# A fused attention and two-layer MoE kernel on one core: logits with the weights held, output additions spread, last pairs' steps in order of tiles, new banks and queues at the start of the second MoE

## The reference

```python
# attention: B=2, H=8, S=576, D=64; the 32 largest scores of each row count
scores = scale * q @ k.T
mask = scores >= kth_largest(scores, 32)
x = softmax(where(mask, scores, -1e9)) @ v          # 1152 tokens x 512
# first MoE: E=8 experts, F=1024, all experts on all tokens, Sinkhorn gates
P = exp(x @ w_gate - max)
for _ in range(8):
    P /= P.sum(1); P /= P.sum(0); P *= N / E
out = sum(P[:, e:e+1] * (relu(x @ w1[e]) @ w2[e]) for e in range(8))
# second MoE, dense: F=2048
h = out @ w_in
g = h * tanh(softplus(h))
result = g @ w_out
```

## Time and profile before

| | |
|---|---|
| three runs | 1254.61, 1255.6, 1258.02 us |
| median | 1255.6 us |
| profiled execution | 1254.9 us, span 1252.8 us |
| granted TensorE clock, mean | 0.985 |
| PE busy | 1202.7 us, 96% |
| DVE busy | 894.3 us, 71% |
| ACT, POOL busy | 685.1 us, 643.1 us |
| DMA | 112 MB, 89 GB/s |

### The profile page before, as it was taken

One profiled execution on the slowest core, in us unless ns is written; L12 is line 12 of the kernel. 1 busy time (PEld: TensorE's weight loads), 2 busy tenths in 40 slices (PEclk: granted clock), 3 DMA queues, 4 the chain that ended last, 5 costly groups with the idle time before them and its releaser, 6 DMA issues.

```text
span 1252.8 us, 19662 instructions
## 1 busy us (share of the span) xinstructions
PE 1202.7 (96%) x6715; PEld 1073.9 (86%) x6715; DVE 894.3 (71%) x1556; ACT 685.1 (55%) x1223; POOL 643.1 (51%) x393
## 2 busy tenths in 40 slices
PE   4878999999999999999999999999999998999998
PEld 4777889999999999998878888888888887898776
DVE  6999998899999940356575464646464647887876
ACT  5667776676777753442243333333333336878776
POOL 1867865556665567753487666666666630000000
PEclk8699999999999999999999999999999999999999
DMA  9034332233223322332233222222222122222230
GB/s 168 9 100 144 120 102 92 94 109 102 94 92 110 110 89 98 118 113 81 68 106 105 68 92 67 90 69 85 74 77 81 44 76 68 68 68 85 85 126 34
DMA packets 150486, 112.10 MB, mean 89 GB/s; under 512 B 34832, under 2 KB 124944, under 8 KB 150416
## 3 DMA queue, kind: packets, MB, share of 16 engines
q1 hardware_dynamic: 150416, 111.19, 29.2%
HBM read 104.09 MB, written 7.08 MB: 89 GB/s over the span
## 4 chain that ended last, share of the span: by engine, by line
PE 78%; DVE 11%; ACT 7%; issue 2%; POOL 1%; DMA 0%; DVEq 0%; SPq 0%; POOLq 0%; ACTq 0%
PE ps L725 15%; PE ps L897 15%; PE ps L739 14%; PE ps L958 14%; PE ps L634 4%; PE ps L1075 4%; PE ps L1053 4%; PE ps L605 3%; PE ps L615 2%; DVE work L1461 2%; DVE top L1459 2%; ACT m_r L1393 1%; ACT m_d L1390 1%; PE ps L594 1%; ACT m_r L1395 1%
## 5 line engine op out<-in xcount | busy, mean ns | idle before, releaser
L1858 POOL TENSOR_TENSOR w_lo<-w_raw,w_hi 128x1024 fp32r<-128x1024 f32 x90 | 218.7, 2431 | 117.4 <-ACT w_hi L1105 117.3
L1105 ACT ACTIVATE w_hi<-w_raw 128x1024 fp32r<-128x1024 f32 (+1 forms) x172 | 179.4, 1044 | 1.6 <-PE ps L897 1.0
L1459 DVE MAX8 top<-work 128x8 f32<-128x576 f32 x216 | 152.2, 745 | 0.0
L725 PE MATMUL ps<-x_hi,w_hi 128*128 128x384 f32 (+3 forms) x384 | 129.5, 337 | 1.7 <-DVE h_lo L1572 1.7
L725 PE MATMUL ps<-x_hi,w_lo 128*128 128x384 f32 (+3 forms) x384 | 128.7, 335 | 0.0
L725 PE MATMUL ps<-x_lo,w_hi 128*128 128x384 f32 (+3 forms) x384 | 128.5, 335 | 0.0
L1865 POOL TENSOR_TENSOR ha_lo<-h_f,ha_hi 128x384 fp32r<-128x384 f32 (+1 forms) x72 | 71.9, 998 | 93.9 <-ACT ha_hi L1182 93.9
L897 PE MATMUL ps<-w_hi,h_lo 128*128 128x512 f32 x296 | 117.2, 396 | 0.0
L897 PE MATMUL ps<-w_lo,h_hi 128*128 128x512 f32 x296 | 117.0, 395 | 0.0
L897 PE MATMUL ps<-w_hi,h_hi 128*128 128x512 f32 x296 | 115.2, 389 | 0.0
L1461 DVE MATCH_REPLACE8 work<-top,work 128x576 f32<-128x576 f32 x144 | 105.7, 741 | 0.0
(11 more groups left out here) (183 smaller groups left out, 3292.4 us busy)
## 6 DMA issues: line engine op xcount, KB each, us to landing
w_raw<-in_moe_w SPq DMA_DIRECT2D x288, 256.0 KB, 3.0
w_raw<-in_moe_w_in SPq DMA_DIRECT2D x32, 256.0 KB, 2.7
w_raw<-in_moe_w_out SPq DMA_DIRECT2D x32, 256.0 KB, 3.0
spill<-y_out SPq DMA_DIRECT2D x5, 768.0 KB, 3.8
y_in<-spill SPq DMA_DIRECT2D x5, 768.0 KB, 4.4
q_parts<-in_q SPq DMA_DIRECT2D x18, 128.0 KB, 3.2
vones<-in_v SPq DMA_DIRECT2D x8, 256.0 KB, 4.9
out<-acc SPq DMA_DIRECT2D x8, 256.0 KB, 2.6
```

Source lines behind the costliest of these rows:

```text
L725: last = nc.tensor.matmul(ps[:, bank, 0:w], wt[:, s, 0, c * P:(c + 1) * P], xt[:, c, token:token + w], start=(n == 0), stop=(n == len(term ...
L1105: return nc.scalar.activation(dst, src, ACT.Copy)
L1459: last = v_.max(top[:, b, op // 2, :], src)
L1858: g_.tensor_tensor(w_lo[:, s, :, :].rearrange("p a n -> p (a n)"), w_raw[:, s, :, :].rearrange("p a n -> p (a n)"), w_hi[:, s, :, :].rearr ...
```

## The change

At the end of the second pass the last round's first unit is clipped and put through ACT one round earlier, and `down2` waits for the low half of each unit only where its first tile needs it. The diff, cut to its core:

```diff
-        X2_BANKS = [HB_BANK, HB_BANK + 1, HB_BANK] + [YB_BANK + t for t in range(PASSES[0] - BLK)]
-        Y2_BANKS = ((2, 3, 4, 5, 6), (7, 2, 3, 4))
+        X2_BANKS = [HB_BANK + 1, HB_BANK, HB_BANK + 1] + [YB_BANK + t for t in range(PASSES[0] - BLK)]
+        Y2_BANKS = ((2, 3, 5, 6, 7), (4, 2, 3, 5))
-        LOGIT_CHUNKS = -(-NT * DC * 2 // (3 * DC + 3 * BLK))
+        LOGIT_CHUNKS = 2
+            if k == 0:
+                return [(2 * F, 0, 0, BT), (2 * F + 1, BT, BT, PASSES[0] * P - BT)]
-        H2_BANKS = (HB_BANK, HB_BANK + 1, 7)
+        H2_BANKS = (HB_BANK, HB_BANK + 1, YB_BANK + BLK - 1)
@@ PE
             def logits():
-                for t in range(NT):
-                    for c in range(DC):
-                        for x in (x_hi, x_lo):
-                            last = nc.tensor.matmul(ps[:, S_BANK, t * GW:(t + 1) * GW],
-                                                    x[:, c, t * P:(t + 1) * P], wg[:, c, :],
...
-                            yield
+                for g in range(NT // BLK):
+                    terms = [(x, c) for c in range(DC) for x in (x_hi, x_lo)]
+                    for n, (x, c) in enumerate(terms):
+                        last = nc.tensor.matmul(ps[0:GW, LOGIT_BANKS[g], 0:BT], wg[:, c, :],
+                                                x[:, c, g * BT:(g + 1) * BT],
...
+            next_chunk(LOGITS, logits)
+            next_chunk(LOGITS + 1, logits_transposed)
@@ PE, down_pair
-                in_order = isinstance(e, int) and (e, p) == (E - 1, NP - 1)
+                in_order = p == NP - 1
@@ PE, last pair
-            x2_transposed(0)
             x2_transposed(1)
-            for n, _ in enumerate(down_pair(E - 1, NP - 1)):
+            for n, _ in enumerate(down_pair(E - 1, NP - 1), start=1):
+                if n == steps_down // 4:
+                    x2_transposed(2)
                 if n == steps_down // 2:
-                    x2_transposed(2)
+                    pe.wait_ge(x2_split, BLK)
+                    up2_unit(0, u0, token0, width0)
+                    x2_transposed(3)
+                    x2_transposed(4)
+                if n == steps_down // 4 * 3:
+                    pe.wait_ge(x2_split, PASSES[0])
+                    up2_unit(0, u1, token1, width1)
@@ ACT, second MoE
+                if F == 2 * NF2 - 2:
+                    first_inverse(u_0, width_0)
@@ DVE, plain chunks
-                if i == ITERS:
-                    add_last_a()
+                if ITERS <= i < ITERS + 3:
+                    add_last_a(i - ITERS)
@@ DVE, hidden_pair
+                if not begin:
+                    for i in range(BLK):
+                        add(i)
                 dve.wait_ge(prod, PRODUCTS * g + 5)
                 v_.tensor_tensor(h22, even, u3, ALU.add).then_inc(c_done, 1)
                 v_.tensor_tensor(u2, even, u2, ALU.add).then_inc(s2_done, 1)
-                add(0)
-                if not (begin and p == 0):
-                    add(1)
@@ DVE, second MoE
+                if F == 2 * NF2 - 2:
+                    u, token, at, w = units_of(F + 1)[0]
+                    clipped(u, w)
@@ POOL
-            for step in range(BC0 + AHEAD, PLAIN):
+            for step in range(BC0 + AHEAD, PLAIN - 1):
                 split_lo(step, step % RING)
             weight_sums(FROM, 0)
+            split_lo(PLAIN - 1, (PLAIN - 1) % RING)
```

More of the change, by code:

```diff
@@ L719, in first_keys, with up @@
                     queries_transposed(0, 3)
-            def up(s, token, w, bank, ready, small=iter(())):
+            def up(s, token, w, bank, ready):
                 terms = [(wt, xt, c) for c in range(DC) for wt, xt in ((w_hi, x_hi), (w_hi, x_lo), (w_lo, x_hi))]
@@ L729, in up, with down @@
                         last.then_inc(ready, 1)
-                    next(small, None)
-            def down(s, hidden, tiles, bank, first, final, bank_read, small=iter(())):
+            def down(s, hidden, tiles, bank, first, final, bank_read):
                 hi, lo = hidden
@@ L760, in down_first, with up_a @@
                                  start=(f == 0), stop=(f == NF - 1)).then_inc(first_used, 1)
-            def up_a(e, f, small=iter(())):
+            def up_a(e, f):
                 if isinstance(e, int) and e == 0:
@@ L1017, in x2_transposed, with up2_unit @@
                 last.then_inc(x2_tr, 1)
+            def up2_unit(F, u, token, w):
+                pe.wait_ge(w_lo_done, M0 + F + 1 + RING)
+                bank_free("unit", u)
+                terms = [(wt, xt, c) for c in range(DC) for wt, xt in ((w_hi, x_hi), (w_hi, x_lo), (w_lo, x_hi))]
+                for n, (wt, xt, c) in enumerate(terms):
+                    last = nc.tensor.matmul(ps[:, h2_bank(u), 0:w], wt[:, F % RING, 0, c * P:(c + 1) * P],
+                                            xt[:, c, token:token + w], start=(n == 0), stop=(n == len(terms) - 1))
+                last.then_inc(h2_ready, 1)
             up_bc(0, 0)
@@ L1035, in _ @@
                 products(E - 1, p + 1, down_pair(E - 1, p), steps_down)
+            (u0, token0, _, width0), (u1, token1, _, width1) = units_of(0)
+            pe.wait_ge(c_done, 4 * PAIRS - 1)
+            x2_transposed(0)
             pe.wait_ge(c_done, 4 * PAIRS)
-            x2_transposed(0)
             x2_transposed(1)
-            for n, _ in enumerate(down_pair(E - 1, NP - 1)):
+            for n, _ in enumerate(down_pair(E - 1, NP - 1), start=1):
+                if n == steps_down // 4:
+                    x2_transposed(2)
                 if n == steps_down // 2:
-                    x2_transposed(2)
[L1042 to L1054, removed]
-                last.then_inc(h2_ready, 1)
+                    pe.wait_ge(x2_split, BLK)
[5 more added lines that the diff above has]
+                    up2_unit(0, u1, token1, width1)
             def up2(F):
@@ L1362, in _ @@
                 hidden_pair(E - 1, p, following=p < NP - 1)
-            for f in range(AHEAD):
-                split_hi(M0 + f, f, RAW + M0 // RING + 1)
             def x2_high(t):
@@ L1639, in hidden_pair @@
                 low(2, 1, 1, h22)
[L1640 removed]
+                if begin:
+                    add(0)
                     add(1)
[L1642 to L1644 removed]
                 dve.wait_ge(prod, PRODUCTS * g + 7)
@@ L1649, in hidden_pair @@
                 low(4, 1, 0, u2)
-                if begin and p == 0:
-                    add(2)
-                    add(3)
-                else:
-                    add(4)
-                    add(5)
+                for i in (2, 3) if begin else (3, 4, 5):
+                    add(i)
                 if p == 1:
```

202 lines of the change are left out of this document (115 added, 87 removed).

## The result

| | before | after |
|---|---|---|
| median | 1255.53 us (4 runs) | 1240.6 us (4 runs) |
| range | 1254.61 to 1258.02 | 1239.24 to 1242.88 |
| ratio | | 0.988, 95% interval 0.9857 to 0.9902 |
| profiled execution | 1254.9, span 1252.8 | 1242.88, span 1241.0 |
| granted clock, mean | 0.985 | 0.983 |

The account below looks back on a forecast made before the run. PE, busy 1202.7 of 1252.8 us, was taken as the bound. 2.9 + 1.8 + 2.2 + 2.3 + 0.7 + 3.5 + 1.4 = 14.8 off 1254.9 gave 1240.1, adjusted towards the median to 1240.5 us; range 1237.5 to 1247.5.

Parts of the forecast that it names:

- Part 1, logits: Logits chunks: 24 matmuls over 384 columns and nine transposes replace 72 small matmuls, 8.1 − 5.2 = −2.9 us.
- Part 2, additions: Plain chunks: nine additions spread three to a chunk fit, so PE's stop goes; −1.8 us, bounds −1.8 and 0.
- Part 2, POOL: Change to pairs: weight sums ahead of POOL's split bring both low parts up to 2.6 us sooner; −2.2 us.
- Part 3, borders: Five borders between experts: PE's 0.47 us wait for the sum of L1647 goes at each; −2.3 us, bounds −2.3 and +1.
- product 7: Borders: behind three additions and two sums, 3.2 us against PE's 4.1, it holds by 0.9.
- Part 3, expert 2: Expert 2's first pair: a 0.55 us wait goes, one addition fewer ahead of the sum; −0.7 us, bounds 0 and −0.7.
- Part 4: Start of the second MoE: units 0 and 1 among the down steps cut losses from 7.2 to 3.7; −3.5 us.
- Part 5: End: the last round's first unit enters the chain a round sooner, 0.1 of 1.5 us stays; −1.4 us.
- B: Rival, chance 0.1: the spread work meets POOL in every chunk and part 2's stops come back; 1244.5 us.
- A: Rival, chance 0.2: the second MoE's start gives nothing back; 1244.0 us, 1245.6 with another fall of the clock.
- C: Rival, chance 0.04: the new logits are no cheaper, matmuls at four times the pitch; 1252.7 us.
- D: Rival, chance 0.03: DVE becomes the bound of the first pass, slower than before; 1264 us.

Follow-up runs that it names:

- logits_only: The kernel before with the logits' new form and two logits chunks instead of four: 1252.83 us against 1255.73, ratio 0.9974.
- pairs_only: The kernel before with the down steps of every expert's last pair in order of tiles and the additions placed to match: 1253.81 us, ratio 0.9987.
- pool_only: The kernel before with POOL's sums of the weights ahead of its last plain split, nothing else: 1254.23 us, ratio 0.9992.
- adds_only: The kernel before with the last nine output additions of part A spread over three chunks, three each: 1254.74 us, ratio 0.9999.
- units_behind: The changed kernel with the two units of round 0 behind the last down steps instead of among them: 1244.28 us.
- units_320: The changed kernel with two equal units of 320 tokens in the first pass: 1240.87 us.

## Why the prediction was right

The time, 1240.6 against 1240.5, owes something to luck. Two sizes were wrong in opposite ways, and the median stands in the middle of a gap between two runs at 1239.2 and 1239.4 and two at 1241.8 and 1242.9. The stages say more.

- **Part 1, logits.** −2.9 forecast, −2.90 in `logits_only`. The price was taken from the nearest row, the pitch at 384 columns, and the weights' width doesn't change it. Nine small transposes took 0.72 us, and about 0.95 with the slow starts around them, where 1.1 was forecast: the four chunks take 21.85 us now, less 4 × 4.18 and 24 × 0.174. The Trainium skill, TensorE: Matmul & The Clock Gate, section "Part 4: PE-mode transpose", has some 275 ns for one in a kernel. The prediction set 0.13 us against that and called it a disagreement; that reading was wrong. One transpose of the kernel before takes 273 ns from its start to its end, as the page has it (count, busy us, mean ns of one):

```profile
L1015 PE MATMUL ps<-ident,acc 128*128 128x128 f32 x36 | 5.1, 273 | 0.4 <-DVE m_a L1750 0.4
```

  In a row they overlap and stand 0.11 us apart, (1.03 − 0.27) / 7 by the earlier trace rows. Their cost in a queue is this distance, not the duration.
- **Part 2, additions.** −1.8 forecast, −1.92 measured. The price of a meeting was right too, 4.21, and so was the argument that a chunk has room for it.
- **Part 2, POOL.** −2.2 forecast. The step "the change runs the sums ahead of the split, so both parts come up to 2.6 sooner" fails as a cause: by itself that gives 1.25, as POOL then waits for ACT. The full change gets all of it, 0.57 + 1.88 and 0.11 twice for the slow first matmuls = 2.7. It moves ACT's split and the x sums too, and I had left out the first and put the second at 0. The wait was 0.32 us at L1890 before, a sign that ACT was next in line.
- **Part 3, borders.** −2.3 forecast, −2.39 measured; product 7 held.
- **Part 3, expert 2.** −0.7 forecast, with "one addition fewer ahead of the sum". This is wrong: before, the first addition stood ahead of product 6's sum and the second behind the low half; now both stand between that low half and the last sum. The order of the queue says it plainly, and I had only counted. These are the rows, two before and one after:

```profile
656.92 0.44 PE L958 MATMUL ps<-x_hi,t_hi 128*128 128x384 f32 x1 [0.22 <-DVE m_r L1629]
662.61 0.44 PE L958 MATMUL ps<-x_hi,w_hi 128*128 128x384 f32 x1 [0.55 <-DVE m_r L1647]
```

```profile
658.23 0.45 PE L964 MATMUL ps<-x_hi,w_hi 128*128 128x384 f32 x1 [0.88 <-DVE m_r L1672]
```

  The stops went from 0.38 and 0.72 to one of 1.04, so with the slow first matmuls 0.2 is gained, and alone the part loses 0.67. The full change comes off better than `pairs_only`, with the stop at 1.04 instead of 1.37; which of its other parts does that was not tried.
- These two errors, 0.5 too little for POOL and 0.5 too much for expert 2, cancel in the sum, and nearly so in the stage: −2.26 against −2.3.
- **Part 4.** −3.5 forecast, −3.53 measured, with both stops at their place and size. Walking two in-order queues with durations of the trace is what gave it; busy shares or the old stops don't say where a new one comes. One entry of the account was no cost of its own, though. I put 1.6 us down to the clock, which fell to 0.51 behind the first stop. `pool_only` has the same code in this stretch and the same stop of 1.80, at 1043.61, and there the clock stays at 1.00 in the 3.5 us at the same place behind it:

```profile
1043.73:1047.23 3.50, 3.44 (x23) 3.20 (x24) 2.67 (x6) 1.42 (x4) 0.00 (x0) 1.00 0.24 83
```

  Its matmuls keep their pitch through the whole stage, and PE stands longer at the next stop, 2.58 instead of 1.31. The waits of L1053 are these instead of the earlier trace rows:

```profile
PE ps L1053 <- DVE m_a L1750: 5.3, 4, 2.6
```

  In `adds_only` the clock holds behind the first stop too and falls behind the second, of 2.58, at 1048.47:

```profile
1048.59:1052.09 3.50, 3.50 (x14) 3.46 (x15) 2.96 (x7) 2.33 (x6) 0.00 (x0) 0.54 0.00 0
```

  A fall behind the first stop, behind the second or none at all: the stage is 58.11, 58.12 and 58.11 us long. What a slow clock takes there, the later waits give back, since DVE and ACT set the pace. The forecast survived because 7.2 and 3.7 are each all that PE loses in the stage, however it is shared between clock and waits.
- **Part 5.** −1.4 forecast, −1.53 in the stage, 1.41 when undone.
- **Rivals.** B's condition came true without its consequence, as said. A is out by the stage and by `units_behind`; C by `logits_only`; D by PE's timeline, which shows no wait between 1055.24 and 1163, through the rest of the first pass.

## What to carry to other kernels

Compare traces by the distance between the same two instructions, and write each term of a forecast for one such stage; effects of 0.5 us can be seen that way where medians of ten runs can't. Where a wait ends on an in-order queue, look for who is next in line at that place on every engine before the whole stop is booked as gain. A stop of the busiest engine in a stretch bound by a chain isn't mended by giving it other work: first shorten the chain, then reorder. Time lost to a slow clock in such a stretch isn't a gain to be booked either.

## What the runs showed that was not expected

**The start of a run.** The changed kernel's profiled execution reached the logits 3.2 us later than before's, in code that is the same. In all other kernels here, changed queues or not, they start within 1 us of before's. From 30 to 70 us the granted clock was 0.61, and PE did 170 matmuls there. The first row is of the changed kernel, the second of before, with 189 at 0.74; the other twelve kernels had 183 to 196 at 0.70 to 0.83:

```profile
30.00:70.00 40.00, 33.43 (x170) 31.23 (x170) 36.19 (x76) 25.67 (x54) 29.76 (x21) 0.61 0.16 44
```

```profile
30.00:70.00 40.00, 32.16 (x189) 29.58 (x190) 38.15 (x81) 27.90 (x60) 31.36 (x23) 0.74 0.16 46
```

The changed kernel's four spans were 1241.0 and 1239.9 us at a mean clock of 0.983 and 0.982, and 1237.5 and 1237.3 at 0.990. Without the 3.2 us the profiled span would be 1237.8, like the last two. That the second run had a late start too is likely but not shown: only one execution has a trace, and the mean clock doesn't tell, since `units_behind` had 0.982 and reached the logits as early as before. What decides it was not tried.

**A stop and the clock.** PE standing 2.26 us at 1041.62 left the granted clock at 1.00 in the 4 us behind; in the kernel before one of 1.80 was followed by 0.51, and in `units_320` one of 2.44 by this:

```profile
1038.25:1042.00 3.75, 3.75 (x14) 3.67 (x15) 3.05 (x6) 2.58 (x6) 0.00 (x0) 0.54 0.02 4
```

The same code with the same stop goes either way as well: 1.80 was followed by 0.51 in before and by 1.00 in `pool_only` and `adds_only`, and 2.58 by 0.54 in `adds_only` and by 1.00 in `pool_only`. So the length of one stop doesn't tell whether the clock falls behind it, and no kernel here was made to find out what does.
